# Attention, a top-2 expert layer and a dense layer in one kernel: the routing of the first 12 token tiles placed inside the attention, logits computed token by token

## The reference, cut to what matters

```python
# q, k, v: (4 batches, 8 heads, 576, 64); tau = 0.02
scores = q @ k.T / sqrt(64)
scores = where(scores >= rowmax(scores) - tau, scores, -1e9)
x = softmax(scores) @ v              # -> tokens (2304, 512), a batch's 8 heads side by side

# expert layer: 8 experts, 512 -> 1024 -> 512
logits = x @ w_gate
noisy  = logits + log1p(exp(x @ w_noise)) * noise
top2, weights = two largest of noisy per token, softmax over the two
out[token] += weight * relu(x[token] @ w1[e]) @ w2[e]     # for both experts e of the token

# dense layer: 512 -> 2048 -> 512, h = max(h, 0) + alpha * min(h, 0) between
```

## Time and profile before

| | us |
|---|---|
| median of 3 runs | 1314.23 (1314.17 to 1314.41) |
| the profiled execution | 1315.53 |
| its span | 1313.8 |

### The profile page before, as it was taken

The page is one execution under the profiler, slowest core; times in us unless marked ns, Lnnn a source line. Parts: engine busy times, 40 slices in busy tenths (PEclk is TensorE's granted clock), DMA queues, the critical chain, the costliest instruction groups (busy, mean ns, idle before and its releaser), DMA issues.

```text
span 1313.8 us, 20231 instructions
## 1 busy us (share of the span) xinstructions
PE 1244.9 (95%) x7678; PEld 1135.9 (86%) x7678; DVE 622.8 (47%) x1249; ACT 539.4 (41%) x966; POOL 568.8 (43%) x412
## 2 busy tenths in 40 slices
PE   5999999999885999999999999998999999999998
PEld 4899999989864889989999999997999999999997
DVE  7888888888745521212212121215544535444433
ACT  5777787878742243333333333333212112112111
POOL 5989999989810344343524434454511101000000
PEclk9999999999986999999999999999999999999999
DMA  5545454453520143343424333344221102000000
GB/s 174 129 120 139 125 148 125 128 135 100 168 52 25 57 153 111 130 129 96 132 93 144 101 123 125 105 161 128 82 73 49 32 1 73 16 0 24 16 1 25
DMA packets 71170, 123.14 MB, mean 94 GB/s; under 512 B 11824, under 2 KB 30512, under 8 KB 71088
## 3 DMA queue, kind: packets, MB, share of 16 engines
q1 hardware_dynamic: 57216, 86.90, 23.4%
q0 software_dynamic: 6080, 19.93, 4.9%
q10 hardware_dynamic: 7792, 15.21, 3.1%
HBM read 82.43 MB, written 19.92 MB: 78 GB/s over the span
## 4 chain that ended last, share of the span: by engine, by line
PE 79%; POOL 6%; issue 5%; ACT 4%; DVE 3%; DMA 2%; SPq 0%; ACTq 0%; POOLq 0%
PE h_ps L702 32%; PE y_ps L721 11%; PE y_ps L720 11%; PE y_ps L719 11%; PE o_acc L560 5%; POOL probs_lo L1311 4%; PE ring L530 2%; PE ring L531 2%; PE t_ps L680 2%; PE ring L544 2%; PE ring L543 2%; POOL k_parts L1316 1%; DMA k_parts<-k_ones 1%; ACT q_hi L805 1%; ACT probs_hi L797 1%
## 5 line engine op out<-in xcount | busy, mean ns | idle before, releaser
L702 PE MATMUL h_ps<-x_hi,region_a 128*128 128x384 f32 (+1 forms) x1408 | 343.8, 317 | 4.8 <-DVE x_lo L1203 4.3
L702 PEld LDWEIGHTS h_ps<-x_hi,region_a 128*128 128x128 f32 x1408 | 246.5, 189 | 11.6 <-DVE x_lo L1203 5.2
L1311 POOL TENSOR_TENSOR probs_lo<-probs,probs_hi 128x576 fp32r<-128x576 f32 x160 | 226.6, 1427 | 34.0 <-ACT probs_hi L797 34.0
L702 PE MATMUL h_ps<-x_lo,region_a 128*128 128x384 f32 (+1 forms) x704 | 221.2, 314 | 0.0
L1213 DVE SCALAR_TENSOR_TENSOR h_lo<-h_ps,h_hi 128x256 fp32r<-128x256 f32 (+1 forms) x128 | 62.8, 491 | 311.6 <-ACT h_hi L896 288.4
L899 ACT ACTIVATE h_hi<-act_out 128x384 fp32r<-128x384 f32 (+1 forms) x112 | 53.7, 480 | 312.3 <-DVE act_out L1224 305.8
L719 PE MATMUL y_ps<-region_b,h_hi 128*128 128x512 f32 x448 | 175.7, 392 | 1.4 <-DVE h_lo L1230 1.4
L720 PE MATMUL y_ps<-region_b,h_hi 128*128 128x512 f32 x448 | 176.5, 394 | 0.0
L721 PE MATMUL y_ps<-region_b,h_lo 128*128 128x512 f32 x448 | 176.5, 394 | 0.0
L1297 POOL TENSOR_TENSOR region_b<-stage,region_b 128x1024 fp32r<-128x1024 f32 x40 | 95.8, 2399 | 143.5 <-ACT region_b L778 143.4
L896 ACT ACTIVATE h_hi<-h_ps 128x256 fp32r<-128x256 f32 (+1 forms) x128 | 56.0, 437 | 240.2 <-PE h_ps L702 231.9
(11 more groups left out here) (202 smaller groups left out, 2406.3 us busy)
## 6 DMA issues: line engine op xcount, KB each, us to landing
stage<-in_moe_w SPq DMA_DIRECT2D x56, 512.0 KB
qk_raw<-in_qk SPq DMA_DIRECT2D x32, 320.0 KB, 3.4
expert_rows<-rows_out ACTq DMA_DIRECT2D x8, 768.0 KB, 3.9
v_nat<-in_v SPq DMA_DIRECT2D x16, 320.0 KB, 3.6
k_ones<-q_hi SPq DMA_DIRECT2D x30, 160.0 KB, 2.6
q_lo<-k_parts SPq DMA_DIRECT2D x30, 160.0 KB, 2.4
q_hi<-q_hi SPq DMA_DIRECT2D x30, 160.0 KB, 2.4
k_parts<-k_ones SPq DMA_DIRECT2D x30, 160.0 KB, 2.9
```

Source lines behind the costliest of these rows:

```text
L702: mm = pe.matmul(h_ps[:, c % 2, 0:width], wt, x[kind][:, cc, :], start=(n == 0), stop=(n == 3 * C - 1))
L1311: pool.tensor_tensor(probs_lo[:, m % 4, :], probs[:, m % 4, :], probs_hi[:, m % 4, :].bitcast(F32), ALU.subtract).then_inc(lo_done, 1)
```

## The change

Tiles 0 to 11 (12 instead of 13) are routed inside the attention, in six pairs, in heads 21, 23, ..., 31. In slot 5 x head PE transposes both tiles of the pair into one ring place (kind "xt"), ACT copies the high part, DVE subtracts the low part and frees the place; in slot 5 x head + 3 PE computes the logits with the token parts stationary and the 32 columns of the router weights moving, into unused columns of `o_acc`. In the last pair's slot PE waits until DVE has added up the logits (`first_logits_read`). Slot 160 holds the early softplus (`soft_terms(0)`), `negative_part(0)`, `choose(0)` and POOL's `routing_constants`. Behind the attention come `first_expert_rows()` and the six late tiles, with logits of the same form. The counts over all tiles move to step 1 of the first expert (`COUNTS_AT`), `late_choice` behind the first `tile_lo`s, the rest of `late_routing` one step later and closer together, and both tiles of the second round are turned at step 7. `early` shrinks to four raw weight parts, used in turn; the token rows come in loads of two tiles. Several buffers change their place in SBUF.

```diff
     SCALE = float(D) ** -0.5
     TILES = NH * NT
     AHEAD = 8
+    PAIRS = 6
+    FIRST_PAIR_AT = 21
     LAG = 3
 
...
         TURN_AT = {"ex": (1, 3, 5), "ml": (5, 7, 9)}
...
             if ph is ex and isinstance(i, int) and i == 0 and w == 0:
-                at = (FS1 - 2, FS1 - 1)
+                return [(tiles(i, 1) + n, UT[0] + n) for n in range(UT[1])] if c == FS1 - 1 else []
             if c >= nw * fs or (last and w == nw - 1) or f not in at[:UT[(w + 1) % 2]]:
                 return []
...
+        def late_place(k):
+
+            n = k % PT
+            kind, at = (0, n) if n < UT[0] else (1, n - UT[0])
+            return kind, slice(at * P, at * P + P)
...
+        def raw_part(n, layer):
+
+            part = early[:, span(2 * (n % RAW_PARTS) + layer, CH // 2)]
+            return part if layer else part.rearrange("p (c f) -> p c f", c=C)
...
-        numbers = {"s": {}, "st": {}, "om": {}}
+        def pair_at(i, c):
+
+            p = (tile(i, c) // NT - FIRST_PAIR_AT) // 2
+            return p if c % NT == 0 and (tile(i, c) // NT - FIRST_PAIR_AT) % 2 == 0 and 0 <= p < PAIRS else None
+
+        def logits_at(i, c):
+
+            return pair_at(i, c - 3) if c % NT == 3 else None
+
+        numbers = {"s": {}, "st": {}, "xt": {}, "om": {}}
         for n in range(FIRST, LAST):
...
             def load_first_weights(n):
 
                 s = first_w_in[n % 4]
-                sp.dma_start(first_layer_part(early, n), w1[0].rearrange("(c p) f -> p c f", p=P)[:, :, span(n, P)]).then_inc(s, 16)
-                sp.dma_start(second_layer_part(early, n), w2[0, span(n, P), :]).then_inc(s, 16)
+                wait(sp, first_w_lo, 2 * (n - RAW_PARTS) + 2)
+                sp.dma_start(raw_part(n, 0), w1[0].rearrange("(c p) f -> p c f", p=P)[:, :, span(n, P)]).then_inc(s, 16)
+                sp.dma_start(raw_part(n, 1), w2[0, span(n, P), :]).then_inc(s, 16)
...
             xr = x_dram.rearrange("(t p) d -> p t d", p=P)
-            x_early = early[:, :].rearrange("p (t d) -> p t d", d=DM)
+            x_late = early[:, 0:LATE_TILES * DM].rearrange("p (t d) -> p t d", d=DM)
+            late_rows = xr[:, FIRST_TILES:TOK, :]
+
+            def rows_stored(heads):
+
+                for n, s in enumerate(x_out):
+                    wait(sp, s, 32 * ((heads // 2 + 1 - n) // 2))
 
             def slot_and_rows(i, c):
                 slot(i, c)
 
-                for k, (n, heads) in enumerate(((TILES - 8, NH - H), (TILES - 3, NH - 2))):
-                    if isinstance(i, int) and tile(i, c) == n:
-                        for n, s in enumerate(x_out):
-                            sp.wait_ge(s, 32 * ((heads // 2 + 1 - n) // 2))
-                        sp.wait_ge(first_w_lo, 2 * NCH)
-                        src = (slice(0, WHOLE), slice(0, DM)) if k == 0 else (slice(WHOLE, TOK), slice(0, DM - 2 * D))
-                        sp.dma_start(x_early[:, src[0], src[1]], xr[:, src[0], src[1]]).then_inc(x_in[k], 16)
+                p = pair_at(i + (c + 4) // SL, (c + 4) % SL)
+                if p is not None:
+                    rows_stored((((2 * p + 2) * P - 1) // S + 1) * H)
+                    wait(sp, pair_turned, p - 1)
+                    sp.dma_start(x_raw[:, p % 2, :, :], xr[:, 2 * p:2 * p + 2, :]).then_inc(pair_in[p % 2], 16)
+                if tile(i, c) == TILES - 3:
+                    rows_stored(NH - 2)
+                    sp.wait_ge(first_w_lo, 2 * NCH)
+                    sp.dma_start(x_late[:, :, 0:DM - 2 * D], late_rows[:, :, 0:DM - 2 * D]).then_inc(x_in[0], 16)
             slots(sp, slot_and_rows)
 
             sp.wait_ge(freed, past("om", 0, NH + 1))
-            for s in x_out:
-                sp.wait_ge(s, 8 * NH)
-            sp.dma_start(x_early[:, WHOLE:TOK, DM - 2 * D:DM], xr[:, WHOLE:TOK, DM - 2 * D:DM]).then_inc(x_in[2], 16)
+            rows_stored(NH)
+            sp.dma_start(x_late[:, :, DM - 2 * D:DM], late_rows[:, :, DM - 2 * D:DM]).then_inc(x_in[1], 16)
...
+                p = pair_at(i, c)
+                if p is not None:
+                    place_free(pe, "xt", 0, p)
+                    pe.wait_ge(pair_in[p % 2], p // 2 * 16 + 16)
+                    for a in range(2):
+                        for cc in range(C):
+                            mm = pe.transpose(ring[:, place("xt", 0, p), a, cc * P:cc * P + P], x_raw[:, p % 2, a, cc * P:cc * P + P], ident[:, :])
+                    mm.then_inc(pair_turned, 1)
...
+                    p = logits_at(i, c)
+                    if p is not None:
+                        pe.wait_ge(freed, past("xt", 0, p))
+                        pe.wait_ge(w_parts_lo, 1)
+                        for a in range(2):
+                            for cc in range(C):
+                                for n, part in enumerate((xt_hi, xt_lo)):
+                                    mm = pe.matmul(o_acc[:, a, HALF + p * 4 * E:HALF + (p + 1) * 4 * E], part[:, a, cc * P:cc * P + P],
+                                                   w_parts[:, cc, :], start=(cc == 0 and n == 0), stop=(cc == C - 1 and n == 1))
+                        mm.then_inc(pair_logits, 1)
+                        if p == PAIRS - 1:
+                            pe.wait_ge(first_logits_read, 2)
...
             pe.wait_ge(mask_ready, 1)
             pe.matmul(first_ps[:, 0:FIRST_TILES], before[:, :], mask_bf[:, 0:FIRST_TILES, 0], start=True, stop=False)
...
             mm.then_inc(first_summed, 1)
...
+            def turn_late(k):
+
+                if k == 0:
+                    for s in x_in:
+                        pe.wait_ge(s, 16)
+                wait(pe, x_lo_r, k - 3)
+                for cc in range(C):
+                    mm = pe.transpose(late_turned[k % 4][:, cc * P:cc * P + P], x_late[:, k, cc * P:cc * P + P], ident[:, :])
+                mm.then_inc(x_turned_r, 1)
+
+            def logits_late(k):
+
+                pe.wait_ge(x_lo_r, k + 1)
+                kind, at = late_place(k)
+                for cc in range(C):
+                    for n, part in enumerate((x_hi, x_lo)):
+                        mm = pe.matmul(late_logits_ps[:, k * 4 * E:(k + 1) * 4 * E], part[kind][:, cc, at], w_parts[:, cc, :],
+                                       start=(cc == 0 and n == 0), stop=(cc == C - 1 and n == 1))
+                mm.then_inc(logits_ready, 1)
+
+            for k in range(LATE_TILES + 4):
+                if k >= 4:
+                    logits_late(k - 4)
+                if k < LATE_TILES:
+                    turn_late(k)
+
+            def count_all():
+
+                pe.wait_ge(mask_ready, 2)
+                flat_mask = mask_bf[:, :, :].rearrange("p t e -> p (t e)")
+                pe.matmul(counts_ps[:, 0:TOK * E], before[:, :], flat_mask, start=True, stop=False)
+                for d in range(1, TOK):
+                    mm = pe.matmul(counts_ps[:, d * E:TOK * E], ones_bf[:, :], flat_mask[:, 0:(TOK - d) * E],
+                                   start=False, stop=(d == TOK - 1))
+                mm.then_inc(counted, 1)
 
...
+                    if ph is ex and isinstance(i, int) and i == 0 and c == COUNTS_AT:
+                        count_all()
                     if ph is ex and isinstance(i, int) and i == 0 and c == SLOTS_AT:
                         sum_slots()
...
+                p = pair_at(i, c)
+                if p is not None:
+                    act.wait_ge(pair_turned, p + 1)
+                    wait(act, pair_logits, p)
+                    act.activation(xt_hi[:, :, :], ring[:, place("xt", 0, p), :, :], ACT.Copy).then_inc(pair_hi, 1)
...
+            def soft_terms(n):
+
+                part = (lambda a: a[:, 0:FIRST_TILES, :], lambda a: a[:, FIRST_TILES:TOK, :])[n]
                 act.wait_ge(route_step, n + 1)
                 act.activation(part(small["exp"]), part(small["neg"]), ACT.Exp).then_inc(route_act, 1)
                 act.wait_ge(route_act, 2 * n + 1)
                 act.activation(part(small["log"]), part(small["exp"]), ACT.Ln, bias=1.0).then_inc(route_act, 1)
...
+                if isinstance(i, int) and tile(i, c) == TILES - 14 * NT:
+                    act.wait_ge(route_in, 48)
+                    act.activation(w_parts[:, :, 0:2 * E], w_logits[:, :, :], ACT.Copy).then_inc(w_parts_hi, 1)
+                if tile(i, c) == TILES:
+                    soft_terms(0)
...
-                    if ph is ex and isinstance(i, int) and i == 0 and c == 1:
+                    if ph is ex and isinstance(i, int) and i == 0 and c == 2:
                         token_rows()
...
+                    soft_terms(1)
                 run_units(act, ph, units)
...
+                p = pair_at(i, c)
+                if p is not None:
+                    dve.wait_ge(pair_hi, p + 1)
+                    dve.tensor_tensor(xt_lo[:, :, :], ring[:, place("xt", 0, p), :, :], xt_hi[:, :, :].bitcast(F32), ALU.subtract)\
+                       .then_inc(freed, 1)
+                if logits_at(i, c) == PAIRS - 1:
```

(59 more changed lines are left out.)

176 lines of the change are left out of this document (50 added, 126 removed).

## The result

The changed kernel took 1327.93 us (median of 4 runs, 1326.1 to 1332.14) against 1314.32 for the kernel before on the same chip (1314.17 to 1314.6): ratio 1.0108, 95% interval 1.0084 to 1.0132, so 13.6 us slower where 4.3 faster was forecast, and outside the range. The profiled execution is the slowest of the four, 1332.14 us with a span of 1330.1; its row can be set beside those of before (span 1313.8), but some of what follows is larger in it than in the median.

What follows compares the result with a forecast made beforehand. TensorE was taken to bound the heads, routing the 52.1 us behind attention. Pairs and drain +18.0, routing before division +7.0, that stretch down to 20.7, +0.7, +1.4: −4.3 us, so 1309.9 against the 1314.23 median; range 1302 to 1319.

Steps and rivals of the forecast that it cites:

- The pair, 2.5 us of TensorE and 0.5 at the ring place: In attention, each added pair costs 3.0 us, TensorE work plus a wait for its ring place; five pairs cost 15.
- Rival 1: In attention, the ring place makes each pair block TensorE through its own chain: 5.7 us a pair, 1323 us; chance 0.20.
- "I take nothing" for the loads: In attention, six 512 KB token row loads on SP, issued four steps ahead, cost nothing; landing has about 3 us margin.
- Its own fallback, 1.4 us a pair: In attention, the loads cost up to 1.4 us a pair if the cover of their landing margin goes.
- The clock in attention: In the heads, pairs were priced with transposes at full clock; no loss from a falling clock was counted there.
- The drain, +3: At attention's end, the sixth pair makes the last probs_lo come 3 us later, bounds 1 and 6.
- Routing ahead of the division, +7: After the last probs_lo, early routing put ahead of the last division adds 7.0 us, division ending at 391.1.
- Division to late tiles, 7.2: Behind attention, the last division takes 0.9 us, then store and reload 6.25, with 3.3 to land, until 397.35.
- Late stage, 14.45: Six late tiles and 3 expert tiles before the first expert matmul take 14.45 us, the clock rising after 9.5 us.
- rival 3: The clock stays low through the late tiles into the first expert: 18.0 us for 14.45, total 1313 to 1316; chance 0.14.
- The row of 366 us: In the kernel before, the clock rose about 9.5 us after work beginning at 366.09, taken as the late stage's model.
- Sums and second round, +2.1: In the expert layer, later slot sums lose 0.7 us in the first expert, two turned tiles 1.4 in the second round.

Runs made afterwards that it cites:

- experiment 11: Experiment 1 with the pairs' logits matmuls moving 128 columns instead of 32, true logits kept: 1309.78 us, ratio 0.9956 to the kernel before.
- experiment 3: The changed kernel without any of the six pairs' work in attention, first 12 tiles' logits zero: 1293.35 us, ratio 0.9836 to the kernel before.
- experiment 1: The changed kernel with each pair's raw row load issued eight slots ahead instead of four: 1319.04 us, ratio 1.0028 to the kernel before.
- experiment 2: The changed kernel without the pairs' logits matmuls and drain reductions, early logits zero; transposes, copies, subtractions stay: 1305.0 us, ratio 0.9922 to the kernel before.
- experiment 5: Experiment 1 with pair matmuls moving 128 columns of other data instead of 32, results unused, early logits zero: 1312.69 us, ratio 0.9972 to the kernel before.
- experiment 4: The changed kernel with the last head's division ahead of the early softplus and choice on VectorE: 1328.63 us, ratio 1.0097 to the kernel before.
- experiment 6: Experiment 1 with pairs in heads 19 to 29 instead of 21 to 31, none in the drain: 1315.84 us, ratio 1.0 to the kernel before.
- experiment 7: Experiment 1 with 34 unread 512-column matmuls filling TensorE's waits behind attention: 1318.59 us, ratio 1.0024 to the kernel before.
- experiment 8: Experiment 1 with the 12 tiles one by one in heads 20 to 31 instead of six pairs: 1311.5 us, ratio 0.9966 to the kernel before.
- experiment 9: Experiment 8 with logits matmuls moving 128 columns instead of 32, in attention and the late stage: 1307.35 us, ratio 0.993 to the kernel before.
- experiment 10: Experiment 9 with 43 unread 512-column matmuls filling TensorE's waits behind attention: 1306.11 us, ratio 0.993 to the kernel before.

## Why the prediction was wrong

**The pair, 2.5 us of TensorE and 0.5 at the ring place: right.** Transposes 0.84, matmuls 0.11 apart (1.8), 3.1 a pair on average in experiment 11 (2.5 to 3.7, each two heads against experiment 3). The Trainium skill (TensorE: Matmul & The Clock Gate, LDWEIGHTS) has the time of a weight load as its columns over 1.2 per ns, by estimate 0.107 us here. The trace agrees with its 0.11, at 32 and at 128 moving columns nearly alike (0.111 and 0.113 to 0.115). Rival 1 had nearly the size for the pairs as made (28.15 us for heads 20 and 21 is 6.7 over before) but not the cause: experiment 1 changed nothing at the ring place and brought heads 22 and 23 to 2.6 over experiment 3. The 0.5 at the ring place is a remainder, not measured by itself, and its own times (3.8 less 2.7) left 1.1 and not 0.5.

**"I take nothing" for the loads: failed.** The load stood behind q_lo's copy on SP, and that copy is held until 245.29. The forecast named the neighbours in the queue but took their idle margin for the new load's. Its own fallback, 1.4 us a pair, was the size of the waits seen (6.3 over the first four pairs), and each also holds up ScalarE's and VectorE's queues. Cost in the medians: 10.0 us, from the change to experiment 1, with some of the clock's scatter in it (experiment 1's interval is ±4.6 us).

**The clock in attention, taken for granted: failed.** The earlier trace rows were read as "low after gaps, high in dense work", and the 16 matmuls were dense, so no term stood for it. Experiments 1, 2, 5 and 11 show that this work itself lowers it: with it 0.87 to 0.96 in two or all of the three stretches of 40 us, without it 1.00, with more moving columns 1.00. In the five profiled kernels with narrow pairs (the change, experiments 1, 4, 6 and 7) a fall begins in the block or up to 1.4 us behind it at 21 of 30 pairs. With wide pairs (5 and 11) it does so at none of the first ten, and at both of the sixth ones in the drain. From experiment 1 to 11 it is 9.8 us: in the profiled executions 4.5 by the last division (397.25 and 392.77) and 6.9 in the late stage (19.3 and 12.45), less 1.0 behind it, where the dense layer is 1.6 longer (410.0 and 408.4).

**The drain, +3: low by 1.6.** 4.6 in experiment 11, with a fall of the clock behind the sixth pair in it; what share of the 1.6 is the clock's stays open.

**Routing ahead of the division, +7: right in size.** 6.8: from the last probs_lo's end to the division 8.9 us, before 2.2. Experiment 4 shows that the order delays the division by that much, but that only 2.4 of it reach the late tiles; the rest is the early routing's own chain.

**Division to late tiles, 7.2 by the forecast's own times: 7.7.** The last columns' load is now 384 KB and landed in 3.7 us, not 3.3. The gathers and first rows were hidden, as forecast.

**Late stage, 14.45: failed, 19.3.** The clock never rose in it, which was rival 3, and that rival's price of 18.0 was low. The row of 366 us was taken for "the same kind of work", but the logits' matmuls of the kernel before move 384 and 256 columns there, not 32. With narrow ones the stage took 19.3 us where the clock stayed low (the change, experiments 1, 4 and 6), 16.2 or 16.3 where it rose and fell again (2, 3 and 5), and 13.6 and 13.1 in experiments 7 and 8; with wide ones 13.7, 11.6 and 12.45 (experiments 9 to 11). The forecast's 14.45 was the size for a clock that rises and stays. It also took 8.25 us of work at full clock, half of its 16.5, where its own count was 8.8; with that it is 15.0. A smaller misreading is the rise in the first expert before, which comes 5.2 us behind its first matmul, not 4.5 (0.66 in 422 to 424).

**Sums and second round, +2.1:** two waits of 1.4 to 1.5 came; the sums ended 0.9 sooner and not 0.7 later. To the dense layer it is +1.7, near the forecast, with the first 3.7 us still at the lower clock (5.2 before). All behind the first expert matmul together is −2.8, so 4.9 better than forecast, and 4.4 of that is the dense layer, for which the forecast had no term.

Set against the profiled spans: +16.3 measured, −4.3 forecast, 20.6 apart; +20.2 by the last division (45.2 for 25), +0.5 to the late tiles, +4.9 in the late stage, −4.9 behind. With the medians, 17.9 apart: 10.0 for the load and 9.8 for the clock, less 1.9 by which experiment 11 beat the forecast, which is luck: the dense layer gave it 2.8. What share of the 10.0 is clock and not waiting stays open; in the profiled executions, by the estimate under experiment 1, it is about half.

## What to carry to other kernels

A load put into an in-order queue arrives when the one ahead of it lets go: look up when its neighbours were issued, not how idle the queue is, and give it a step or two more. Work that is added to a busy matrix engine has a second price beside its length, what it does to the clock of what follows; a block of matmuls that moves few columns for each weight load should be suspected, and if the load sets its pace anyway, moving more columns costs next to nothing (0.113 to 0.115 us a matmul for 0.111). When a kernel's runs scatter and their times follow the mean clock, mend that first: other differences can't be read under it. And compare the stages that a change leaves alone as well: here one of them moved by as much as the whole gain that was forecast.
